# Splitting the first value transfers over two queues and moving the late tiles by one pair

## The reference

```python
X = np.fft.rfft(x, axis=1)
Yr = Xr @ w_r - Xi @ w_i + b_r
Yi = Xr @ w_i + Xi @ w_r + b_i
Yr = np.sign(Yr) * np.maximum(np.abs(Yr) - lam, 0.0)   # Yi likewise
y = np.fft.irfft(Yr + 1j * Yi, n=x.shape[1], axis=1)
h = x @ w_in
x = (np.maximum(h, 0.0) + alpha * np.minimum(h, 0.0)) @ w_out      # layer 1; layer 2 likewise, other function
```

## Time and profile before

| | |
|---|---|
| median of 3 runs | 1165.75 us (1165.38 to 1167.25) |
| profiled execution | 1165.22 us, span 1163.4 us |
| TensorE busy | 1155.2 us, 99% of the span, granted clock 1.00 in every slice |
| VectorE, ScalarE, GpSimd busy | 76%, 75%, 59% |
| DMA, first four slices (29 us each) | 9, 9, 8, 9 tenths busy; 318, 380, 284, 278 GB/s |
| median landing of a store of `a_sb` / of values | 5.4 us / 4.9 us |

### The profile page before, as it was taken

One profiled execution on the slowest core, in us unless ns is written; L12 is line 12 of the kernel. 1 busy time (PEld: TensorE's weight loads), 2 busy tenths in 40 slices (PEclk: granted clock), 3 DMA queues, 4 the chain that ended last, 5 costly groups with the idle time before them and its releaser, 6 DMA issues.

```text
span 1163.4 us, 20900 instructions
## 1 busy us (share of the span) xinstructions
PE 1155.2 (99%) x6982; PEld 1118.3 (96%) x6982; DVE 879.6 (76%) x1583; ACT 868.5 (75%) x1881; POOL 685.3 (59%) x714
## 2 busy tenths in 40 slices
PE   8999999999999999999999999999999999999998
PEld 3788899999999999999999999999999999999998
DVE  4777777677777777777778787878788787878765
ACT  3567777777776777777767788888888887878776
POOL 0027557676666666666556566665656575757553
PEclk9999999999999999999999999999999999999999
DMA  9989312012020211102005400000000000000000
GB/s 318 380 284 278 110 29 68 28 59 78 29 68 29 75 52 64 42 29 68 19 33 199 167 2 1 28 1 28 1 28 1 27 2 27 1 28 1 18 11 28
DMA packets 41164, 79.69 MB, mean 68 GB/s; under 512 B 4576, under 2 KB 20960, under 8 KB 40288
## 3 DMA queue, kind: packets, MB, share of 16 engines
q1 hardware_dynamic: 38480, 68.52, 17.6%
q10 hardware_dynamic: 2576, 9.82, 2.2%
HBM read 48.05 MB, written 30.28 MB: 67 GB/s over the span
## 4 chain that ended last, share of the span: by engine, by line
PE 67%; DVE 0%; issue 0%
PE bank L1396 36%; PE bank L1304 31%; PE bank L1289 1%; DVE u L1062 0%; DVE y_tile L1116 0%
## 5 line engine op out<-in xcount | busy, mean ns | idle before, releaser
L578 POOL TENSOR_TENSOR g_lo<-g_sb,g_hi 128x376 fp32r<-128x376 f32 x510 | 506.8, 1005 | 363.6 <-ACT g_hi L861 362.9
L1396 PE MATMUL bank<-g_hi,w_out_lo 128*128 128x376 f32 x1024 | 342.9, 335 | 0.0
L1396 PE MATMUL bank<-g_hi,w_out_hi 128*128 128x376 f32 x1024 | 342.4, 334 | 0.0
L1304 PE MATMUL bank<-xc_hi,w_in_hi 128*128 128x376 f32 x896 | 302.4, 338 | 0.0
L1304 PE MATMUL bank<-xc_hi,w_in_lo 128*128 128x376 f32 x896 | 300.3, 335 | 0.0
L1304 PE MATMUL bank<-xc_lo,w_in_hi 128*128 128x376 f32 x896 | 298.6, 333 | 0.0
L861 ACT ACTIVATE g_hi<-g_sb 128x376 fp32r<-128x376 f32 x512 | 261.1, 510 | 46.2 <-DVE g_sb L1094 28.8
L1396 PE MATMUL bank<-g_lo,w_out_hi 128*128 128x376 f32 x1024 | 259.8, 335 | 0.0
L1396 PEld LDWEIGHTS bank<-g_hi,w_out_hi 128*128 128x128 f32 x1024 | 192.5, 188 | 0.8
L1396 PEld LDWEIGHTS bank<-g_hi,w_out_lo 128*128 128x128 f32 x1024 | 192.3, 188 | 0.0
L1396 PEld LDWEIGHTS bank<-g_lo,w_out_hi 128*128 128x128 f32 x1024 | 184.7, 188 | 0.0
(11 more groups left out here) (94 smaller groups left out, 1454.8 us busy)
## 6 DMA issues: line engine op xcount, KB each, us to landing
gc<-group_consts SPq DMA_DIRECT2D x24, 256.0 KB, 5.0
slots_scratch<-a_sb ACTq DMA_DIRECT2D x24, 256.0 KB, 5.4
inverse_scratch<-v_sb SPq DMA_DIRECT2D x24, 256.0 KB, 3.9
ut<-inverse_scratch SPq DMA_DIRECT2D x16, 384.0 KB, 4.7
out<-y_tile SPq DMA_DIRECT2D x30, 188.0 KB, 1.9
zt<-slots_scratch SPq DMA_DIRECT2D x21, 256.0 KB, 4.9
x_sb<-x SPq DMA_DIRECT2D x10, 512.0 KB, 8.8
prep_raw<-wpack SPq DMA_DIRECT2D x16, 256.0 KB, 2.6
```

The costliest lines, as they stand in the source:

```text
L578: pool.tensor_tensor(g_lo[kind][:, :], g_sb[n % 3][:, :], g_hi[kind][:, :].bitcast(f32), ALU.subtract)\
L1304: done = pe.matmul(bank_of[:, 0:N], w_part[:, fp, w * P:(w + 1) * P], x_part[q % 2][:, xs, :], start=first and n == 0, stop=last_one and n ...
L1396: last = pe.matmul(acc_bank[k][c][:, 0:N], w[:, fp, upper * D + c * P:upper * D + (c + 1) * P], g_part[kind][:, :], start=first and n == 0 ...
```

## The change

The four transfers of the first two pairs' values are issued by both engines: SyncE issues the two with c = 0, ScalarE the two with c = 1, behind its first two copies of the mixing matrices and ahead of the third. Matrices 1 are now issued behind both of SyncE's value transfers. SyncE waits for forward(1) before it loads tile 9 and matrices 3; tile 10 and those after it move one step later in its loop. Tiles 9 to 15 are transformed one pair later, and their stores are spread anew. The filler product behind tile 8 and the longer one behind forward(0) go.

```diff
-LATE_TILES = {2: 9, 3: 10, 4: 11, 5: 12, 6: 13, 7: 14, 8: 15}
-LATE_STORES = {0: ((0, 1), (2, 1)), 1: ((4, 1), (6, 1)), 2: ((0, 2), (2, 2)), 3: ((4, 2), (6, 2)),
-               4: ((8, 0), (8, 1)), 5: ((8, 2), (10, 0)), 6: ((10, 1), (10, 2)), 7: ((12, 0), (12, 1)), 8: ((12, 2),),
-               9: ((14, 0), (14, 1), (14, 2))}
+LATE_TILES = {3: 9, 4: 10, 5: 11, 6: 12, 7: 13, 8: 14, 9: 15}
+LATE_STORES = {0: ((0, 1), (2, 1)), 1: ((4, 1), (6, 1)), 3: ((0, 2), (2, 2)), 4: ((4, 2), (6, 2)),
+               5: ((8, 0), (8, 1)), 6: ((8, 2),), 7: ((10, 0), (10, 1)), 8: ((10, 2),),
+               9: ((12, 0), (12, 1)), 10: ((12, 2), (14, 0)), 11: ((14, 1), (14, 2))}
...
-WAIT_PRODUCTS = {TILES_PER_BATCH - 1: 6 * (512,), TILES_PER_BATCH: (512,)}
-FORWARD_PRODUCTS = (512, 256)
+WAIT_PRODUCTS = {TILES_PER_BATCH - 1: 6 * (512,)}
+FORWARD_PRODUCTS = (256,)
...
+        def load_first_values(eng, half, c):
+            groups = slice(2 * half, 2 * half + 2)
+            eng.dma_start(zt[0][c:P:2, groups, :], az_quads[0][0, c, 0, :, groups, :])\
+               .then_inc(zt_in[0] if half else zt_first_in, 16)
...
-            load_first_values(0)
+            load_first_values(sp, 0, 0)
+            load_first_values(sp, 1, 0)
             load_matrices(1)
-            load_first_values(1)
             load_values(1, (0,))
             load_matrices(2)
+            sp.wait_ge(b_done, 2)
             load_x(sp, 9)
             load_matrices(3)
-            load_x(sp, 10)
...
-                if p + 10 < TILES:
-                    load_x(sp, p + 10)
+                if p + 9 < TILES:
+                    load_x(sp, p + 9)
...
                     act.activation(wm_hi[:, X_SUM, :], wm_raw[:, 0, :], ACT.Copy).then_inc(wm_hi_ready, 1)
+                    act.wait_ge(a_stored[0][0], 16 * (TILES_PER_BATCH // 2 - 1))
+                    act.wait_ge(a_last_stored, 16)
+                    load_first_values(act, 0, 1)
+                    load_first_values(act, 1, 1)
                     act.wait_ge(wm_both_ready, 2)
                     act.activation(wm_hi[:, X_RE, :], wm_both[:, X_RE, :], ACT.Copy).then_inc(wm_hi_ready, 1)
...
-            act.wait_ge(a_stored[0][0], 16 * (TILES_PER_BATCH // 2 - 1))
-            act.wait_ge(a_last_stored, 16)
             act.dma_start(zt[1][1:P:2, :, :], az_quads[0][0, 1, 1, :, :, :]).then_inc(zt_in[1], 16)
```

More of the change, by code:

```diff
@@ L400, in load_values @@
                       .then_inc(zt_in[n % QUAD_SLOTS], 16)
[L402 to L406, removed]
             def store_pair(p):
```

## The result

| | before | changed |
|---|---|---|
| median of 13 runs | 1165.78 us (1165.0 to 1167.25) | 1168.64 us (1166.7 to 1171.14) |
| ratio to before | | 1.0026, 95% interval 1.0017 to 1.0034 |
| profiled execution, span | 1165.22 us, 1163.4 us | 1169.43 us, 1167.6 us |

What follows compares the result with a forecast made beforehand. TensorE, busy 99%, was taken as the bound. Start -1.1 plus hole at pairs 11 and 12 +2.5 gave +1.4 us: 1166.6 on the profiled execution, 1167.1 as median; forecast range 1165.8 to 1168.0, wide range 1164.5 to 1169.6.

Steps and rivals of the forecast that it cites:

- (a): Start: ScalarE issues transfer 2 at about 18.8, so forward(0) starts at 21.85, 0.7 us earlier; bounds 0.86 and 0.2.
- (b): Start: forward(1), needing transfers 3 and 4 and matrices 1, starts at 23.4, 2.1 us earlier.
- (c): Start: the ScalarE and VectorE chain limits the gain; first split of pair 1 at 25.55, mix(1) 1.1 us earlier, at 29.1.
- Rival 3: Start doesn't move because ScalarE's halves land late and forward(0) gains 0.2 or loses 0.25: +2.4, 1168.1 us; chance 0.10.
- (d): Forward(2): matrices 2 land at 27.9, before the 28.1 needed, so no cost; 0.3 us if 0.5 later.
- (f): Forward(4): values of quad 2, which wait for pair 1's stores, cost 0; bound 0.9 us.
- (e): SyncE's new wait for forward(1) delays matrices 3; they land at 31.4, before forward(3) at 32.5: no stall, bound 0.5 us.
- (g): ScalarE's third matrix copy about 1.5 us later costs nothing; two fillers gone, 1.28 us of products, ran in waiting time.
- (h): Pair 11: ScalarE's first weight copy waits for its own just-issued stores, landing in 4.5 at 81.55; TensorE loses 2.5 us.
- (i): SyncE step 9: later part 0 store delays matrices 12; forward(12) 1.6 us late, bounds 0.1 and 4.7, inside ScalarE's larger hole.
- Rival 2: Pair 11: ScalarE's store lands in 5.4 or more, hole 3.4 to 4.8, about 1168.8 us; chance 0.20.
- rival 4: Start: clock falls to 1.2 GHz with fillers gone and TensorE waiting, +3.1 on top of the forecast, 1170.2 us; chance 0.03.

Runs made afterwards that it cites:

- matrices first: Changed kernel with matrices 12, inverse result and raw weights ahead of SyncE's wait for the part 0 store in step 9: 1170.65 us, ratio 1.0039.
- both waits treated: Changed kernel with all three stores of tiles 14 and 15 at pair 10 and matrices 12 ahead of SyncE's wait: 1165.78 us, ratio 0.9997.
- start alone: Changed kernel with the tile and store tables of the kernel before, so only the new start remains: 1165.88 us, ratio 0.9997.
- late tiles only: Kernel before with the changed tile and store tables and tile loads one step later, start as before: 1170.11 us, ratio 1.0039.
- ScalarE's wait only: Kernel before with the stores of parts 1 and 2 of tiles 14 and 15 at pair 11 instead of 9: 1172.08 us, ratio 1.0054.
- hole filled: Changed kernel with five 256-column filler products ahead of forward(12), where TensorE stands: 1169.18 us, ratio 1.0028.
- matrices 1 between: New start with the old tile tables, matrices 1 issued between SyncE's two value transfers: 1165.20 us, ratio 0.9996.

## Why the prediction came out as it did

- (a) F(0) at 21.85: measured 21.83. The gain is real, but the hit to 0.02 is luck. The last transfer was SyncE's first (18.79 + 3.0 = 21.79), not ScalarE's, which landed in 2.6. Over the profiles the mean of F(0) goes from 22.9 (four, start as before) to 22.0 (six, as changed).
- (b) failed: F(1) at 23.4, measured 25.93. The prediction gave each transfer the landing of its neighbour before (3.0 to 4.0). ScalarE's second transfer went at 20.0, not 19.45 (its two issues took 1.59), and landed in 5.7, matrices 1 in 5.6. Over the same profiles the mean of F(1) is 25.6 with either start: what F(0) gains is gone by F(1). Which transfer is the last differs between profiles; that issuing them closer together lengthens their landings fits this and is not tested by itself.
- (c) was right as a bound, but did not act: ScalarE's first split of pair 1 went at 27.10, 1.2 behind F(1), not 25.55. mix(1) stood 0.58 for the sum of parts. The start term of -1.1 was +0.4 in the profile and 0.0 in the medians. Rival 3 (the start doesn't move) is what happened in the sum; its reason, a late F(0), is not.
- (d), (f) no stall, as said. (e) held in the changed kernel; its bound of 0.5 was too small: with the same list F(3) stood 0.93 for matrices 3 in the kernel with matrices first and 0.37 in the one with both waits treated. In (g) the two fillers that go are 0.85 each by the rows, 1.7 together and not 1.28; nothing hangs on it.
- (h) the mechanism and its formula were right: wait 4.58, landing 4.8 against 4.5. In the changed kernel alone the wait is covered by (i), which the prediction held to be the smaller. Rival 2's 1168.8 is the nearest number of all by luck: its condition, a landing of 5.4 or more, wasn't met.
- (i) was mis-sized: part 0 landed in 2.3 (said 2.9), but matrices 12 in 5.3 (said 3.7), so F(12) was 2.3 late, not 1.6, and this was the hole that counted. (The upper bound of 4.7 should be 4.3: 72.65 + 3.9 + 1.75 + 5.4 - 79.43.) (h) with L = 82.17 less 0.43 gives 2.7, a wait of 0.4 more, which shows as such only when the clock is kept up.
- The clock stood as rival 4, at the start of the kernel and with 0.03. There it did fall in the profile of the start alone. In the changed kernel's it fell behind the hole of (i) instead and cost 1.5 in that execution. The prediction had a hole of 2.5 us in hand and gave it no clock term; in the kernel before no hole was longer than 0.5.

So the forecast of +1.4 was made of -1.1 and +2.5; the profile has +0.4, +2.3 and +1.5, the medians +2.9 of which the start has none that shows. The hole had about the size of the forecast by another of its two waits; the time is above the forecast by the missing gain of the start and, where it fell, by the clock, and the range held it because it was 5 us wide. The Trainium skill (DMA: Bandwidth & Descriptors, Latency and other measured facts) says that a lighter load makes the fixed cost smaller. The landings of ScalarE's second store go that way: 2.4 with SyncE silent, 4.8 and 6.5 with three and eight of its transfers issued just ahead. But more than a fixed cost is in them: from 77.5 to 78.5 in the changed kernel 1 of 250 packets was of ScalarE's queue, while both of its stores waited.

## What to carry to other kernels

Before a store is moved later, look for every wait on its semaphore and on which engine's list it stands: a wait on a transfer that the same engine has just issued stalls all that is queued behind it for a whole landing, and it cost 6 us here by one table entry (4.4 of it the wait and 1.2 the clock in the profile). Price a moved transfer by the traffic that it will meet and by the spread of its landings, not by the one landing it had; and give a hole like the ones here (2.2 us and more on TensorE) a term for the half clock behind it, which cost 1.2 and 1.5 where it was read. Look at where the profiled execution stands among the others before reading a hole as typical. Where one code gives starts that differ by a microsecond, compare several profiles.

## What was not expected of the hardware

- The granted clock fell to half behind standings of 2.22, 2.25 and 2.50 us (changed, late tiles only, start only) and of 3.76 us (ScalarE's wait only). It stayed at 1.00 behind one of 3.42 us (matrices first) and behind 2.51 us ahead of F(1) in the changed kernel. The length alone doesn't decide.
- A store of 256 KB from ScalarE around 68 to 78 us took 2.3 to 6.5 us. What SyncE had issued just ahead is a part of it: 2.3 and 2.4 with nothing, 4.6 to 5.4 with three transfers (changed, hole filled, late tiles only), 6.5 with eight. It isn't all: with the same transfers of SyncE ahead, the store of part 0 took 3.9 in the kernel before and 6.5 in the one with matrices 1 between. While the changed kernel's store waited (77.4 to 77.5), all packets in the window were of SyncE's queue.
- ScalarE's two value issues took 1.59 us in its list, SyncE's two 1.33 at the same moment.
